# Expert-layer steps between the pairs of list columns, fewer in the digit levels, and scatters in another order

## The reference

```
x   = irfft(rfft(x, 2S) * rfft(h, 2S))[:, :S]        # long convolution along the sequence
# layer 1: 8 experts, each takes exactly N/8 = 2848 rows
order = argsort(-(x @ w_gate).flatten())             # all (row, expert) pairs, best first
for (row, e) in order:
    if row is free and counts[e] < 2848: assigned[row] = e; counts[e] += 1
out[rows of e] = relu(x[rows of e] @ w1[e]) @ w2[e]  # 128 -> 1024 -> 128
# layer 2: 8 experts, each row goes to its best one
e = argmax(logits2); p = softmax(logits2)[e]
out[row] = p * (relu(x[row] @ w1b[e]) @ w2b[e])
```

## Time and profile before

| | |
|---|---|
| runs, us | 2347.20, 2356.96, 2360.69 |
| the profiled execution's own time | 2342.93 us, span 2341.1 us |
| busy share of the span | PE 84%, DVE 55%, ACT 40%, POOL 31% |
| TensorE clock granted, mean | 0.917 of 2.4 GHz |

### The profile page before, as it was taken

One profiled execution on the slowest core, in us unless ns is written; L12 is line 12 of the kernel. 1 busy time (PEld: TensorE's weight loads), 2 busy tenths in 40 slices (PEclk: granted clock), 3 DMA queues, 4 the chain that ended last, 5 costly groups with the idle time before them and its releaser, 6 DMA issues.

```text
span 2341.1 us, 36407 instructions
## 1 busy us (share of the span) xinstructions
PE 1975.6 (84%) x10729; PEld 1530.3 (65%) x10729; DVE 1284.0 (55%) x4137; ACT 947.6 (40%) x2046; POOL 726.8 (31%) x618
## 2 busy tenths in 40 slices
PE   7886999799634978788887888796959999999998
PEld 3343444355423857566666667584759999999998
DVE  2224777422378756656574756511246666666665
ACT  3334887422111423333332323252425555555554
POOL 0001000000144244352516263446423443434434
PEclk9898999899855999898988989797979999999999
DMA  7776999778783011111101111101168888888885
GB/s 194 258 245 215 312 310 308 200 208 206 212 299 123 19 34 28 36 33 31 35 27 38 33 31 39 45 25 39 32 211 289 276 279 283 276 287 278 280 282 176
DMA packets 161018, 382.35 MB, mean 163 GB/s; under 512 B 29813, under 2 KB 88876, under 8 KB 135581
## 3 DMA queue, kind: packets, MB, share of 16 engines
q1 hardware_dynamic: 120749, 287.59, 39.0%
q10 hardware_dynamic: 11696, 57.94, 7.1%
q0 software_dynamic: 28480, 35.66, 5.4%
HBM read 273.07 MB, written 109.13 MB: 163 GB/s over the span
## 4 chain that ended last, share of the span: by engine, by line
PE 63%; DVE 11%; DMA 9%; issue 8%; another core or an unknown queue 4%; SPq 2%; POOL 2%; ACT 1%; ACTq 0%; DVEq 0%; POOLq 0%
PE bank L842 9%; PE bank L928 8%; PE bank L929 8%; PE bank L930 8%; DMA arena<-in_dft_mid_dram 4%; PE bank L772 3%; PE bank L863 3%; PE bank L751 3%; PE bank L865 3%; PE bank L752 2%; PE bank L864 2%; DMA arena<-in_h_dram 2%; PE bank L672 2%; DVE ge L1371 2%
## 5 line engine op out<-in xcount | busy, mean ns | idle before, releaser
L1131 ACT ACTIVATE arena<-bank 128x356 f32<-128x356 f32 x512 | 237.9, 469 | 557.1 <-PE bank L865 437.7
L842 PE MATMUL bank<-arena 128*128 128x356 f32 x1024 | 416.9, 491 | 1.0 <-issue 0.9
L1528 DVE SCALAR_TENSOR_TENSOR hlo<-bank,hhi 128x374 fp32r<-128x374 f32 x544 | 297.8, 548 | 191.1 <-ACT hhi L1164 138.8
L1657 POOL DMA_INDIRECT out_dram<-orow,slot x204 | 247.0, 1211 | 381.0 <-DVE slot L1567 327.0
L1164 ACT ACTIVATE hhi<-bank 128x374 fp32r<-128x374 f32 x544 | 262.9, 483 | 250.8 <-PE bank L930 211.1
L863 PE MATMUL bank<-xhi,wsp 128*128 128x356 f32 x512 | 281.5, 550 | 18.8 <-issue 9.4
L1634 POOL DMA_INDIRECT sorted<-arena,slot x192 | 205.4, 1070 | 180.3 <-DVE slot L1309 115.2
L1625 POOL DMA_INDIRECT xr<-conv_y,idx x192 | 209.4, 1091 | 153.4 <-PE bank L811 83.8
L928 PE MATMUL bank<-xhi,wsp 128*128 128x374 f32 x544 | 193.1, 355 | 3.6 <-DMA wsp<-w_split 3.6
L842 PEld LDWEIGHTS bank<-arena 128*128 128x128 f32 x1024 | 192.6, 201 | 2.2 <-issue 1.5
L1606 POOL TENSOR_TENSOR wsp<-arena,wsp 128x1024 fp32r<-128x1024 f32 x16 | 41.8, 2614 | 468.5 <-ACT wsp L1081 468.5
(11 more groups left out here) (216 smaller groups left out, 3669.6 us busy)
## 6 DMA issues: line engine op xcount, KB each, us to landing
wsp<-w_split SPq DMA_DIRECT2D x136, 1024.0 KB, 5.4
arena<-spec_a SPq DMA_DIRECT2D x90, 320.0 KB, 3.4
spec_a<-arena ACTq DMA_DIRECT2D x16, 1600.0 KB
spec_b<-arena SPq DMA_DIRECT2D x90, 256.0 KB, 3.6
arena<-spec_b SPq DMA_DIRECT2D x16, 1280.0 KB
arena<-in_dft_mid_dram SPq DMA_DIRECT2D x90, 192.0 KB, 4.3
arena<-in_moe_w_dram SPq DMA_DIRECT2D x32, 512.0 KB, 5.5
w_split<-wsp ACTq DMA_DIRECT2D x16, 1024.0 KB, 6.4
```

The source lines that it names most:

```text
L842: r = mm(bank[Z1[t % 2]][:, 0:T1], w2raw[u][:, f * D:(f + 1) * D], h32[:, f, :], start=(f == 0), stop=(f == FC - 1))
L1131: nc.scalar.activation(h32[:, f, :], bank[H1[q % len(H1)]][:, 0:T1], ACT.Relu).then_inc(m_hh[0], 1)
L1528: v.scalar_tensor_tensor(hl[:, f, 0:T], bank[f % 4][:, 0:T], 0.0, hh.bitcast(F32)[:, f, 0:T], ALU.max, ALU.subtract).then_inc(m_hl[m_], 1)
L1657: nc.gpsimd.indirect_dma_start(out=out[:, :], out_offset=place(slot2[u][0:n, s:s + 1]), in_=orow[3 * u + s][0:n, :], in_offset=None, bound ...
```

## The change

The shares of a stage's 64 places become: 14 ahead of the first count (10 before), 3 and 1 in each level (3 and 2), 6 before `ties` (8), 2 behind `listing_head` (3), and 10 between the 12 pairs of columns (none; the 3 behind them are gone). `listed(g)` tells how many of the 10 stand ahead of pair g. In the last stage, which has no levels, the same 10 stand between its pairs. DVE's share of the steps is called at the same places, and once more at the end of `choose`.

The scatters are put behind other fetches: `after(t)`. Of the 8 tiles t = 0 to 7 (mod 8), 3, 4 and 5 stand behind fetch t+9, and 6, 7 and the 0, 1, 2 of the next eight all behind the last fetch of an expert. The first four fetches of an expert have none behind them. From tile 51 on the order is as before.

For tiles whose `back1` falls in the last 70 steps (`FREE` = step 442), the way back uses bank 6 instead of `X1`, so that it no longer shares a bank with `x_T1`. Batches without a rank point in a level are ranked from step 390 on at the earliest (`rank_step`).

```diff
@@ -88,8 +88,8 @@
 
 SLOT = FC * PER_E
 HEAD = 6
-CHOOSE, LUMP_A, LUMP_B, TIES, LIST = 10, 3, 2, 8, 3
-assert CHOOSE + NL * (LUMP_A + LUMP_B) + TIES + 2 * LIST == SLOT
+CHOOSE, LUMP_A, LUMP_B, TIES, LIST, PAIRS = 14, 3, 1, 6, 2, 10
+assert CHOOSE + NL * (LUMP_A + LUMP_B) + TIES + LIST + PAIRS == SLOT
 STEPS = FC * NT1
 
 
@@ -98,6 +98,11 @@
     if st == 0:
         return 0
     return max(0, SLOT * (st - 1) - HEAD + n)
+
+
+def listed(g):
+
+    return g * PAIRS // (EC // 2)
 
 
 def xT_step(t):
@@ -130,6 +135,11 @@
             if due(st, CHOOSE + (j + 1) * (LUMP_A + LUMP_B)) >= gate_step(i) + 4:
                 return st, j
     return None
+
+
+def rank_step(i):
+
+    return max(gate_step(i) + 3, due(E - 1, LIST + PAIRS))
 
 
 def constants():
@@ -463,6 +473,12 @@
         H1 = (0, 1, 2)
         Z1 = (3, 4)
         X1 = 5
+        FREE = due(E - 1, SLOT)
+
+        def back_bank(t):
+
+            return 6 if back_step(t) >= FREE else X1
+
         CNT = (6, 7)
         SUM, TIE = 6, 7
         RK, TOT = 0, 128
@@ -806,7 +822,8 @@
                 if t >= 1:
                     pe.wait_ge(m_xc[0], t)
                 if t >= 3:
-                    pe.wait_ge(m_zrc, t - 2 if back_step(t - 2) >= xT_step(t) else t - 1)
+                    shared = [k for k in range(t) if back_step(k) < xT_step(t) and back_bank(k) == X1]
+                    pe.wait_ge(m_zrc, len(shared))
                 for s, n in enumerate(SUBS1):
                     last = tp(bank[X1][:, s * P:s * P + n], xr[u][0:n, s, 0:D], ident[0:n, 0:n])
                 last.then_inc(m_xp[0], 1)
@@ -815,9 +832,12 @@
                 pe.wait_ge(m_zc[0], t + 1)
                 if t >= 1:
                     pe.wait_ge(m_zrc, t)
-                pe.wait_ge(m_xc[0], min(NT1, t + 2 if xT_step(t + 2) > back_step(t) else t + 3))
+                if back_bank(t) == X1:
+                    pe.wait_ge(m_xc[0], min(NT1, t + 2 if xT_step(t + 2) > back_step(t) else t + 3))
+                else:
+                    pe.wait_ge(li_gc, EC // 2 * E)
                 for s in range(3):
-                    last = mm(bank[X1][:, s * (D + E):(s + 1) * (D + E)], zT[t % 2][:, s * P:(s + 1) * P], idg[:, :],
+                    last = mm(bank[back_bank(t)][:, s * (D + E):(s + 1) * (D + E)], zT[t % 2][:, s * P:(s + 1) * P], idg[:, :],
                               start=True, stop=True)
                 last.then_inc(m_zr[0], 1)
 
@@ -826,6 +846,8 @@
                 pe.wait_ge(m_oh, i + 1)
                 if i:
                     pe.wait_ge(m_pr, i)
+                if rank_point(i) is None:
+                    pe.wait_ge(li_gc, EC // 2 * E)
                 mm(bank[CNT[1]][:, RK:RK + E * n], tri[:, :], ohb[:, 0:E * n], start=True, stop=True)
                 mm(bank[CNT[1]][:, TOT:TOT + E * n], ones[:, :], ohb[:, 0:E * n].rearrange("p (k e) -> p e k", e=E),
                    start=True, stop=True).then_inc(m_pf, 1)
@@ -866,7 +888,7 @@
                 if q >= LAG:
                     layer2_1(q - LAG)
                 for i in range(NBT):
-                    if rank_point(i) is None and q == gate_step(i) + 3:
+                    if rank_point(i) is None and q == rank_step(i):
                         ranks(i)
 
             def moe1(a, b):
@@ -896,16 +918,17 @@
                 moe1(due(st, at_ + TIES), due(st, at_ + TIES + LIST))
                 for g in range(EC // 2):
                     listing_rows(st, g)
-                moe1(due(st, at_ + TIES + LIST), due(st, SLOT))
+                    moe1(due(st, at_ + TIES + LIST + listed(g)), due(st, at_ + TIES + LIST + listed(g + 1)))
             listing_head(E - 1)
             moe1(due(E - 1, 0), due(E - 1, LIST))
             for g in range(EC // 2):
                 listing_rows(E - 1, g)
-            moe1(due(E - 1, LIST), STEPS)
+                moe1(due(E - 1, LIST + listed(g)), due(E - 1, LIST + listed(g + 1)))
+            moe1(due(E - 1, LIST + PAIRS), STEPS)
             for q in range(STEPS - LAG, STEPS):
                 layer2_1(q)
             for i in range(NBT):
-                if rank_point(i) is None and STEPS <= gate_step(i) + 3 and i < NBT - 1:
+                if rank_point(i) is None and STEPS <= rank_step(i) and i < NBT - 1:
                     ranks(i)
             back1(NT1 - 1)
             ranks(NBT - 1)
@@ -1107,7 +1130,7 @@
 
             def rows_out1(t):
                 i, j = BATCH_OF[t]
-                both = bank[X1][:, 0:3 * (D + E)].rearrange("p (s d) -> p s d", s=3)
+                both = bank[back_bank(t)][:, 0:3 * (D + E)].rearrange("p (s d) -> p s d", s=3)
                 act.wait_ge(m_zr[0], t + 1)
                 if i >= 2:
                     act.wait_ge(m_oh, i - 1)
@@ -1320,7 +1343,7 @@
                             gate_max(i)
                         if q == gate_step(i) + 1:
                             gate_onehot(i)
-                        if q == gate_step(i) + 3 and rank_point(i) is None:
+                        if rank_point(i) is None and q == rank_step(i):
                             gate_place(i)
                 done[0] = max(done[0], to)
 
@@ -1358,6 +1381,7 @@
                 c.then(v.tensor_tensor(hitb[:, :, :], hitb[:, :, :], bc_e(scoreb[:, :]), ALU.mult))
                 c.then(v.tensor_reduce(arg[:, :], hitb[:, :, :], AX, ALU.max))
                 c.then(v.tensor_tensor(arg[:, :], arg[:, :], tmp[:, 0, :], ALU.add))
+                moe1(due(st, CHOOSE))
 
             keybytes = keyi[:, 0, :].bitcast(U8).rearrange("p (c k) -> p c k", k=4)
 
@@ -1410,6 +1434,7 @@
                         c.did(v.tensor_scalar(le[:, kk, :], rows[:, k, 0:NC], tab("slot")[:, kk:kk + 1], 0.0, ALU.is_le, ALU.add,
                                               accum_out=lcnt[:, kk:kk + 1]))
                     v.tensor_copy(lpart[:, 2 * g:2 * g + 2], rows[:, :, NC]).then_inc(li_gc, 1)
+                    moe1(due(s, n + listed(g + 1)))
                     if g % 6 == 5:
                         c.wait()
                         dve.wait_ge(li_gc, EC // 2 * s + g + 1)
@@ -1501,7 +1526,7 @@
             listing(E - 1, LIST)
             moe1(STEPS)
             for i in range(NBT):
-                if gate_step(i) + 3 >= STEPS:
+                if rank_step(i) >= STEPS:
                     if gate_step(i) >= STEPS:
                         gate_max(i)
                     if gate_step(i) + 1 >= STEPS:
@@ -1638,7 +1663,12 @@
             for u in range(2):
                 pool.wait_ge(y_st[u], 32 * (NG // 2))
 
-            after = lambda t: t + (8 if t < PER_E * (E - 2) + 3 else 5)
+            def after(t):
+                if t >= PER_E * (E - 2) + 3:
+                    return t + 5
+                r = (t + 1) % PER_E
+                return t + 9 if r >= GB else t + 8 - r
+
             sends = 0
             for t in range(NT1):
                 if t % PER_E == 0:
```

## The result

| | before | after |
|---|---|---|
| median of 8 runs each, us | 2358.92 (2347.20 to 2364.24) | 2337.43 (2325.57 to 2347.79) |
| the profiled execution, us | 2342.93, span 2341.1 | 2332.93, span 2331.1 |
| TensorE clock granted, mean | 0.917 | 0.919 |

The ratio is 0.9928 with a 95% interval of 0.9907 to 0.9949: the change makes the kernel 21 us faster. The forecast of 2275 us was 82 us under the median that stood beside it, 70 us by its sum, and its range ended at 2325 us. So the sign was right and the size was not.

The account below looks back on a forecast made before the run. PE was taken as the bound, losing some 22 us a stage to waits and some 10 to its lower clock. Terms summing to 70 us off 2342.9 gave 2273 profiled; forecast 2275 us, range 2230 to 2325.

Parts of the forecast that it names:

- The clock's term: Behind the pairs and their head: half of the 4.8 us lost to the lower clock comes back, 17 us gained.
- part 1: Ten steps between the 12 pairs in seven listings: waits shrink, 24 us gained, plus 17 us by the clock.
- part 2: One step less between count and total: 0.5 us for each of 48 levels, 24 us lost.
- part 4: Front of an expert without scatters: second tile's gather wait goes, 15 us gained; late relu event goes, 40 us gained.
- part 5: Back of an expert, 15 scatters behind the last fetch: 4 us for each of six runs, 24 us lost.
- part 6: Last expert: 15 us gained there, 6 for the event after the last listing, 1 for bank 6.
- the bank's 1: Bank 6 for the last ways back frees the turn of a wait of a copy: 1 us gained.
- Part 3: Steps moved to ahead of the first count, from before ties and around the pairs: cost 0, bounds -1 and +1 us a stage.
- The first: Rival: scatters at an expert's end hold up PE's signals, 21.8 us for each of six runs; 2380 us, chance 0.08.
- The event isn't the scatters': Rival: late relus stay in each stage and with the last expert, new runs cost nothing extra; 2304 us, chance 0.18.
- The levels eat it: Rival: each of 48 levels pays the whole step, 60 us instead of 24; 2309 us, chance 0.10.
- POOL is held up: Rival: scatters in the levels slow beside DVE's bf16 work, next gathers 13 us late in five stages; 2338 us, chance 0.04.

Follow-up runs that it names:

- e10: Changed kernel with its ten steps behind the 12 pairs of columns instead of between them; 2233.71 us, 0.9903 of the kernel before (chip 15).
- e8: Changed kernel with scatters spread, three steps between ties and head, and an expert's first gather ahead of the low weights; 2142.64 us, 0.9493 of before (chip 3).
- e5: The changed kernel, no edit, on quick chip 3; 2188.03 us, 0.9701 of the kernel before.
- e6: The kernel before, no edit, one execution on a quick chip for its trace; 2260.57 us.
- e9: Changed kernel with eight steps moved from ahead of the first count to the levels, two between count and total; 2199.72 us, 0.9765 of before (chip 15).
- e13: e8 plus three steps ahead of the last listing's head and the last expert's first send one fetch later; 2238.94 us, 0.9520 of before (chip 4).
- e14: Changed kernel with the way back of all tiles in bank X1, as before the change; 2339.25 us, 0.9929 of the kernel before (chip 4).
- e15: The changed kernel again, no edit, on slow chip 4; 2333.44 us, 0.9914 of the kernel before.

## Why the prediction was wrong in size

Layer 1 split into PE's waits, its busy time, and the part of the busy time at the lower clock, in us (from the same traces; gaps under 0.05 us count as busy):

```
                  waits   busy   of it at the lower clock
before, slow      153.1  798.2   137.6
after, slow       158.7  776.9    94.9
before, quick      90.8  774.1   102.1
after, quick       51.5  741.1    25.4
pairs bare (e10)   72.6  768.9    70.6
all three (e8)     19.7  730.0     9.5
```

The clock's term of the sum was about right: 17 us forecast, for the stretches behind the pairs, and 21 less busy time measured in all of layer 1 on the slow chip and 33 on the quick one. (The mean clock of a stage hides this, since it counts the waits too.) The waits are wrong: all other terms together forecast 53 us less, and on the slow chip they are 5.6 us more. Term by term, gain in us:

| term | forecast | slow | quick |
|---|---|---|---|
| pairs, waits (part 1) | 24 | 31 | 31 |
| one step less in a level (part 2) | -24 | -4 | -4 |
| second gather (part 4) | 15 | 14 | 13 |
| late reports of before go (part 4) | 40 | 42 | 0 |
| late reports in the new order (part 5) | -24 | -83 | 0 |
| last expert and after the last listing (part 6, without the bank's 1) | 21 | 2 | 4 |
| head of the last listing | 0 | -4 | -4 |
| sum | 52 | -2 | 40 |
| measured waits | | -5.6 | 39.3 |

For the slow chip the two rows on late reports are differences to the quick one, and its -4 for the levels is the quick chip's.

**The step that failed** is the price of late reports in the new order. Part 5 ("I take 4 us, nearer to the first ... 24 us lost") was all that the prediction booked for them, and part 4 had them gone from the levels. The two together were to give 40 - 24 = 16 us; they cost 83 - 42 = 41. The 83 us stand in two places. The first is the head behind the 12 scatters: the heads' waits of stages 2 to 6 are 51.9 us where e5 has 21.3, and stage 1's 3.2 more, 34 us. That is 5.6 us a listing, near the 4 taken. The second is the levels, for which the prediction booked nothing: totals cost 9.3 to 10.7 us in each of stages 2 to 6 and 3.7 in stage 1, where e5 has 0.7 and 0.4, 49 us. Of it 28 us stand behind three scatters, three gathers and three scatters in a row, and 12 behind a later run of three and three. The prediction could have read the first from its own trace, which has the same run with relus up to 5.5 us late. What made it dearer, from 2.0 to 2.5 us a stage to 5.0 to 6.4, stays open: the latest report is 0.5 to 2.8 us later, and there is one step less between count and total. So part of the 49 us may belong to part 2.

**Part 4** sized the old event well: stages 2 to 6 wait 109.8 us before on the slow chip and 67.5 in e6, 42 us for 40, and it went from the first levels. It had the reason wrong: the front's run isn't broken up (20.9 us in a row), but it holds no scatters, and gathers alone have no late relu. And in the levels behind it as much was lost again as went.

**Part 2** was too dear on the quick chip. There PE waits ahead of two of a stage's eight totals, up to 0.4 us each: 0.7 us for eight levels instead of 4. On the slow chip its share isn't known.

**Part 1** was too careful: the two pairs with no step ahead wait no longer either (0.3 us in all). e10 shows the whole, waits and clock, as 46 us against 41.

**Part 3** holds: e9 shows that the front's steps hide DVE's choice.

**Part 6** holds on neither chip. The last stage waits 8.0 us less on the slow chip, 4.5 on the quick one, but the event after the last listing stays on the slow chip, up to 12.9 us late near 1544 us, with 5.7 us ahead of ways back; and in both a wait of 3.7 us ahead of the last listing's head is new: that head follows the pairs of the listing before, and where three steps stood between them, one does (e13, with three more there, has no such wait). What the bank gave is open (e14).

**On a quick chip** the sum of the terms that exist there is 40 + 33 = 73 us, and 67 were measured. The forecast's 70 agrees with that by luck: its 40 and its 24 belong to a mechanism that isn't there.

**The rivals.** The first had the mechanism (scatters hold up PE's signals at the end of an expert). There they cost 5.6 us a run against its 21.8; with the levels it is 83 / 6 = 13.8, not far below the 15.7 us a run from which the kernel gets slower. "The event isn't the scatters'" falls as the traces stand: the late reports moved when the scatters did, to the same steps in each measurement of the changed kernel, and grew with their runs. No run on the slow kind moved the scatters alone. "The levels eat it" falls by e5, and on the slow chip by its own sign: two of a stage's eight totals wait over 1 us, not most. "POOL is held up" falls by the mean scatter of 1.01 us.

What the prediction never asked is whether the chip of its profile is like others. It booked 40 us of gain on an event that four of five chips don't have.

## What to carry to other kernels

Steps of independent work between small dependent ones (pairs, a head) pay twice, by the wait and by the clock behind it: on the quick chips 46 us here for ten steps a stage, 34 more for three ahead of the head. Where a trace has consumers that run several us behind a producer's end with no releaser named, don't book their removal as a gain: they can move with the work that you move, so the term needs both its signs. Look through the whole trace for such consumers, not only where the longest wait stands. Measure the kernel before again on other chips before explaining a few per cent.

## What was not expected of the hardware

**Two kinds of chip.** The same kernel takes 2253 to 2256 us on chips 0, 3, 12, 15 and 2355 to 2359 on chip 4 and in the first measurement. Single instructions take the same on both (a scatter 1.01 us, a gather 1.13 in the first trace after; 1.04 a scatter in e5). What differs is that reports of matmuls in layer 1 come late, by up to 12.9 us in the changed kernel and 17.1 in e13.

**Missing records.** Counted over the whole trace, the semaphore events recorded are 21,286 after and 21,877 before in the first measurement and 20,984 to 21,135 in e13 to e15, but 27,904 to 27,922 in each quick run of the same work. What is missing are mostly landings of DMAs that POOL issued (4,300 to 4,800 are recorded instead of 9,400): in 850 to 1500 us the changed kernel has 67 to 175 landings in each 50 us instead of 336 to 544 in e5. Some 700 to 900 of the engines' own events are missing too. So on the slow kind both late and lost records stand beside dense indirect DMAs. That the chip's path for such records is full there, and holds the engines' own signals up, is argued and not shown. The Trainium skill (NOTIFIC — Programmer's Manual, "When the ring fills") says that a full queue of records either loses them or makes the engine stand until there is room. The trace agrees with lost ones by its counts; every run here was recorded with its span and clock, so none shows what the kernel takes without records.

**The clock.** e8's granted clock is 1.00 over stages 2 to 5, with 2.0 to 2.2 us of waits a stage; e6's is 0.91 to 0.94 with 13 to 14 us. Stage 5 is 16.3 us shorter in e8, of which 11.0 are waits; 5.3 are work done at 2.4 instead of 1.2 GHz.
